# Seven loads issued earlier, and two state products put ahead of the outputs, in a delta-rule layer with two feed-forward layers

## The reference, cut to what matters

```python
# q, k, v: (4, 8, 768, 48); beta: (4, 8, 768)
k_n = k / (norm(k) + 1e-6)
for t in range(768):
    y[t]  = q[t] @ state
    v_old = k_n[t] @ state
    state = state + beta[t] * outer(k_n[t], v[t] - v_old)
x = y as (3072, 384)
h = x @ w_in1;  g = piecewise quadratic of h;  x = g @ w_out1    # w_in (384, 2048), w_out (2048, 384)
h = x @ w_in2;  g = relu(h) ** 2;              out = g @ w_out2
```

## Time and profile before

| | |
|---|---|
| profiled execution | 982.77 us, of which the span is 981.0 us |
| median of the three runs | 983.34 us |
| TensorE busy | 964.0 us, 98% of the span |
| VectorE, ScalarE, GpSimd busy | 602.9, 407.5, 41.1 us |
| data moved | 50.72 MB, mean 52 GB/s |
| mean granted TensorE clock | 0.997 |

### The profile page before, as it was taken

The page is one execution under the profiler, slowest core; times in us unless marked ns, Lnnn a source line. Parts: engine busy times, 40 slices in busy tenths (PEclk is TensorE's granted clock), DMA queues, the critical chain, the costliest instruction groups (busy, mean ns, idle before and its releaser), DMA issues.

```text
span 981.0 us, 23854 instructions
## 1 busy us (share of the span) xinstructions
PE 964.0 (98%) x9996; PEld 784.3 (80%) x9996; DVE 602.9 (61%) x1480; ACT 407.5 (42%) x690; POOL 41.1 (4%) x58
## 2 busy tenths in 40 slices
PE   7899999999999999999999999999999999999998
PEld 7688788778877877787778888888888888888887
DVE  6899798787978788788646773433334334333332
ACT  6667543443443433443436553333333333333332
POOL 6710000000000000000000000000000000000000
PEclk9899999999999999999999999999999999999999
DMA  8152240113012200110004411010010010000000
GB/s 273 67 173 66 60 131 35 32 31 93 34 34 69 67 30 26 56 55 2 2 13 161 161 33 65 1 47 18 1 64 1 1 65 1 33 1 1 33 1 33
DMA packets 28842, 50.72 MB, mean 52 GB/s; under 512 B 2368, under 2 KB 17728, under 8 KB 28736
## 3 DMA queue, kind: packets, MB, share of 16 engines
q1 hardware_dynamic: 28736, 49.19, 15.3%
HBM read 39.75 MB, written 9.44 MB: 50 GB/s over the span
## 4 chain that ended last, share of the span: by engine, by line
PE 92%; DVE 3%; ACT 2%; DMA 2%; issue 1%; SPq 1%; DVEq 0%; ACTq 0%
PE psum L1350 39%; PE psum L1326 39%; PE psum L1072 2%; PE psum L1242 2%; PE psum L1158 2%; PE psum L1097 2%; PE psum L1209 1%; PE psum L1216 1%; PE psum L1023 1%; DMA ring<-in_v_s 1%; DVE act_g L1652 1%; DVE tmp L1504 1%; PE psum L1225 1%; PE psum L1173 1%; DVE x_inv L1508 1%
## 5 line engine op out<-in xcount | busy, mean ns | idle before, releaser
L1326 PE MATMUL psum<-x_hi,w 128*128 128x512 f32 x1152 | 390.3, 394 | 0.0
L1350 PE MATMUL psum<-g_hi,w 128*128 128x512 f32 x1152 | 389.9, 394 | 0.0
L1350 PEld LDWEIGHTS psum<-g_hi,w 128*128 128x128 f32 x1152 | 216.1, 188 | 48.5 <-issue 1.8
L1326 PEld LDWEIGHTS psum<-x_hi,w 128*128 128x128 f32 x1152 | 216.0, 188 | 47.8
L1658 DVE TENSOR_TENSOR g_lo<-act_g,g_hi 128x512 fp32r<-128x512 f32 x192 | 132.4, 690 | 172.8 <-ACT g_hi L898 172.5
L1350 PE MATMUL psum<-g_lo,w 128*128 128x512 f32 x576 | 224.2, 389 | 0.0
L1326 PE MATMUL psum<-x_lo,w 128*128 128x512 f32 x576 | 224.0, 389 | 0.0
L898 ACT ACTIVATE g_hi<-act_g 128x512 fp32r<-128x512 f32 x192 | 121.3, 632 | 243.1 <-PE psum L1350 184.3
L1652 DVE TENSOR_TENSOR act_g<-act_g 128x512 f32<-128x512 f32 x96 | 66.4, 692 | 112.1 <-ACT act_g L891 112.1
L1350 PEld LDWEIGHTS psum<-g_lo,w 128*128 128x128 f32 x576 | 108.2, 188 | 21.3
L1326 PEld LDWEIGHTS psum<-x_lo,w 128*128 128x128 f32 x576 | 108.2, 188 | 21.3
(11 more groups left out here) (145 smaller groups left out, 627.1 us busy)
## 6 DMA issues: line engine op xcount, KB each, us to landing
kt_sb<-in_k_t SPq DMA_DIRECT2D x24, 256.0 KB, 4.2
qt_sb<-in_q_t SPq DMA_DIRECT2D x23, 256.0 KB, 3.3
ring<-in_v_s SPq DMA_DIRECT2D x24, 192.0 KB, 2.9
between_layers<-y_out SPq DMA_DIRECT2D x6, 768.0 KB, 3.9
x_sb<-between_layers SPq DMA_DIRECT2D x6, 768.0 KB, 5.6
result<-y_out SPq DMA_DIRECT2D x5, 768.0 KB, 3.9
gram_or_states<-in_k_s SPq DMA_DIRECT2D x15, 192.0 KB, 2.6
wi_st<-in_w_in SPq DMA_DIRECT2D x7, 384.0 KB, 3.6
```

Of the source, the lines that this page charges most:

```text
L1326: ins = pe.matmul(h_ps[n % 2][:, :], w_in_part(layer, f // GW, part)[:, kt, fs], x[:, kt, :], start=(at == 0), stop=(at == len(terms) - 1))
L1350: ins = pe.matmul(acc[kt][:, :], w_out_part(layer, f // GW, part)[:, f % GW, ds], g[n % 2][:, :], start=(f == 0 and j == 0), stop=(f == NF ...
```

## The change

On SyncE's queue, the loads of the keys of chunk 2 (items 8 to 11) and of the queries of items 4 to 6 are moved from behind the weights of group 4 to ahead of the wait for the first four outputs (`y_done` at 4), behind a new wait for the first inverse (`xc_ready` at 1). On TensorE's queue, the state changes of items 6 and 7 are moved ahead of the outputs of items 6 and 7, as it is at f = 14.

```diff
@@ SyncE
             load_weights(0, 2, w_in1, w_out1)
             load_weights(0, EARLY, w_in1, w_out1)
+            sp.wait_ge(xc_ready, 1)
+            for m in range(2 * B, 3 * B):
+                load_kt(m)
+            for m in range(B, B + QUERIES):
+                load_qt(m)
             sp.wait_ge(y_done, B)
             load_qt(EARLY_ITEM)
             for k in range(NB):
                 load_v(k + RING)
             load_weights(0, EARLY + 1, w_in1, w_out1)
-            for m in range(2 * B, 3 * B):
-                load_kt(m)
-            for m in range(B, B + QUERIES):
-                load_qt(m)
             for m in range(B, B + 2):
                 load_kn(m)
@@ TensorE, beside(t, f)
                 m = change_at(t, f)
-                if m is not None and f < NF - 1:
+                if m is not None:
                     state_change(m)
                     state_change(m + 1)
                 m = outputs_at(t, f)
...
                     outputs(m)
                     outputs(m + 1)
-                m = change_at(t, f)
-                if m is not None and f == NF - 1:
-                    state_change(m)
-                    state_change(m + 1)
```

## The result

The changed kernel takes 989.17 us in the median of 11 runs (985.12 to 991.39), the kernel before 983.53 (982.17 to 984.09, 11 runs beside it). The ratio is 1.0056 [1.0042, 1.007], so 4.1 to 6.9 us were lost. I had predicted 983.8 us, and the measured time lies above my whole range.

A forecast was written before the change was run, and what follows sets the result against it. TensorE was taken as the bound, busy 964.0 of 981.0 us. Loads 0, swap 0 and kn wait 0.45 us gave 983.22 us for the profiled execution, 983.8 on the median; range 982.5 to 985.7 us.

The forecast's parts named there:

- the cost of the moved loads: From 38 to about 46 us, beside the first solves: at most 0.1 us by GpSimd's subtraction, taken as 0.
- Rival C: From 38 to 55 us: early loads hold up an instruction fetch, at most 3.7 us, giving 987.5 us; chance 0.06.
- The moved loads gain nothing: First use at 71.47 us, step 4: no wait of TensorE was on these loads, so gain 0.
- Rival D: From 58 to 70 us: the loads had crowded TensorE's operand reads; moving them gives back 2.4 us, 981.4 us; chance 0.06.
- The swap itself costs 0: Step 15: state changes and outputs together take 4.26 us in either order, so cost 0.
- The wait for `kn`: State changes at 139.06 us wait for loads landing 4.2 us after issue at 135.19; loss taken as 0.45 us.
- Rival A: Step 15: the loads for items 6 and 7 land in time, so the time is 983.3 us; chance 0.15.
- B: From 139.06 us: kn lands late, giving 985.7 us at a middle of 2.4 us, 987.5 at most; chance 0.12.
- The cover behind the outputs: Steps 15 and 16: outputs end 1.07 us later relative to TensorE, but 1.15 and 1.4 us of cover remain; cost 0.

The follow-up runs named there:

- e1: Only the seven loads moved as in the change, state changes left in place, against the kernel before: 986.62 us, ratio 1.0036.
- e5: Only the seven loads moved, and 20 instead of 28 small filler products ahead of the first solve, against the kernel before: 990.01 us, ratio 1.0071.
- e4: Only the seven loads moved, issued one by one, each behind one more solved part of the first chunk, against the kernel before: 983.09 us, ratio 1.0004.
- e6: Only the seven loads moved, still earlier, behind the keys-by-queries products of items 0 to 3, against the kernel before: 982.66 us, ratio 0.9999.
- e10: Kernel before, no load moved, TensorE made to wait in the first solve for GpSimd's second low part: 989.36 us, ratio 1.0055.
- e7: Only the four loads of keys moved behind the first inverse, the three of queries left in place, against the kernel before: 983.2 us, ratio 1.0009.
- e3: State changes moved, and kn loads for items 6 and 7 put ahead of the queries' load, against the kernel before: 982.69 us, ratio 1.0.
- e2: Only the state changes of items 6 and 7 moved as in the change, loads left in place, against the kernel before: 983.2 us, ratio 1.0006.
- e9: Kernel before, no load moved, TensorE made to wait in the first solve for GpSimd's first low part: 984.17 us, ratio 1.0025.

## Why the prediction was wrong

**The step that failed** is the cost of the moved loads: "they now run from 38 to about 46 us, beside the short chain of first solves", priced at 0 from GpSimd's subtraction. That row measured how an engine at work fares beside full DMA engines, and TensorE fared well too, as long as it had instructions. The measured price is about 3.5 us by e1's ratio, and 3.9 of the 5.2 us in the two profiles. It has two terms. The first is 1.5 to 2.3 us of late instructions, shown by e5 to be at a position in the instruction stream, and by e4 and e6 to come at this place from the burst. The second is the half clock behind it, shown by e10 to need no DMA traffic at all: 2.17 us in the changed kernel and 1.5 in e1, and 3.4 to 3.6 in e5, e7 and e10. That the moved bytes would be worked through from 38 to about 46 us was right.

**Rival C had the mechanism and a chance of 0.06.** It named the place, the resource and, with 987.5 us, nearly the time. I argued it away with 38 matmuls in one microsecond at a DMA share of 0.81. That microsecond was too short: in the chain the packets of instructions lie about 4 us apart, so a single one can pass without any fetch. The count was at hand, 80 packets and the microseconds in which they lie; read beside the 8 us that the burst would last, it says that one fetch, perhaps two, must fall into it. The same reading offers a reason why the burst at 56 to 70 us did no harm: TensorE takes 5 matmuls a microsecond there, and in the kernel before the packets start at 54.06 and 66.53 us, over 12 us apart, so a late one has more room. No run tested it. C's price of at most 3.7 us was built for one late fetch alone, and left out the clock behind it. The rule that I set beside it was no help: the Trainium skill ("DMA: Bandwidth & Descriptors", Queues, rings and completion order) has a DMA engine take turns between queues packet by packet, by which the fetch would have waited for a packet and not for a backlog. Beside the seven loads the q8 packet came about 3 us late; whether it was requested later or served later, the trace does not show, so the rule itself is neither confirmed nor refuted.

**The moved loads gain nothing**: right. e4 and e6 have them early without the stall and are at 1.0004 and 0.9999. Rival D falls with this: between the first state change and step 14, where the moved loads would have crowded the products, the distance to the kernel before stays at 3.94 us.

**The swap itself costs 0**: right, by e3's 12.83 us.

**The wait for `kn`**: right in place and cause, too small in size. I took 4.2 us from issue to landing and 0.45 us of loss; e2 has 4.33 and 0.78, and the changed kernel 4.64 and 1.08. The second load's own wait is the likely rest: the pair took 1.34 and 1.33 us for 1.07, and 1.07 again in e3, with both loads early. Rival A, the loads in time, is out; B's mechanism is this one, with 1.08 us and not with its 2.4 or more. Why these loads landed in 4.64 us after the change and in 4.2 before it stays open. The fit that I set beside them, 2.6 us, is given by the Trainium skill ("DMA: Bandwidth & Descriptors", Anatomy of one DMA) as measured on transfers that GpSimd issues, and these are SyncE's (for loads of this size the page of the kernel before has medians of 3.3 us for the queries and 4.2 for the keys).

**The cover behind the outputs** was worked out exactly. VectorE after the change, as in the earlier trace rows:

```profile
149.60 1.90 DVE L1631 TENSOR_TENSOR x_lo<-x,x_hi 128x512 fp32r<-128x512 f32 x3 [2.79 <-ACT x_hi L867]
...
152.57 0.69 DVE L1655 TENSOR_TENSOR g_lo<-act_g,g_hi 128x512 fp32r<-128x512 f32 x1
```

x_low ends at 151.50 and first_product(16) starts at 152.65, 1.15 later; g_lo ends at 153.26 and second_product(15) starts at 154.69, 1.43 later. I had 1.15 and 1.4.

**What stays open.** Runs of the changed kernel spread from 985.12 to 991.39 us, those of the kernel before from 982.17 to 984.09. In general the long ones of the changed kernel have the lower mean clock: 985.12 at 1.000, 991.39 at 0.984. So the clock's part differs from run to run, but the profile of one execution can't say by how much in each. Nor is it settled why e5, which differs from e1 by eight spare matmuls, took 3.4 us more than it in the median. For the two profiled executions, 3.9 us apart, the traces say where it went: 2.5 us by the first state change (59.73 against 57.25), 0.4 of it a longer stall and the rest mostly a clock of 0.50 for 10.2 us instead of 3.4, and 1.1 us in e5's second stall at 417.24. Why the clock stayed low for 3.4 us behind one stall and for 10.2 behind a shorter one is open too.

## What to carry to other kernels

Before you put a burst of loads beside a stretch of many small instructions, look where the instruction packets lie in the profile's DMA queues, and compare the time between two packets with the time that the burst will keep the DMA engines full. Where the packets lie closer together than the burst is long, spread the loads out or issue them before the dense stretch. Allow for more than the length of any stall of TensorE on the critical path: here 2.2 us of idle time cost 5.6, because the clock fell behind it, and 1.7 us cost only themselves in six runs of ten.

## What the runs showed of the hardware

- Seven loads of 256 KB issued within 3.2 us came with an instruction packet of 16 KB that started 1.9 to 2.8 us later than in the kernel before, and TensorE stood for 1.47, 1.85 and 2.29 us (e1, e5, the changed kernel); four loads, for 1.01 us in one profiled run (e7); one at a time, for 0.39 us at another place (e4).
- In these stalls TensorE went on 2.2 to 2.7 us after the start of an instruction packet.
- TensorE's granted clock fell from 1.00 to 0.50 about 2 us after the end of the stall in e1 and the changed kernel, and within 0.3 us of it in e5, e7 and e10. It stayed there for 3.4 us (e1), 6.8 us (the changed kernel) and 10.2 us (e5, e7, e10). Behind 1.7 us of waiting it stayed at 1.00 in one profiled execution (e9), behind 1.01 us it fell in another (e7), so the length of the stall alone doesn't decide it.
